# Gate sums taken from the value products: w_gate applied to v, head by head, in place of the transposed output rows

## What is computed

```python
    scores = scale * np.matmul(q, k.transpose(0, 1, 3, 2))      # B=2, H=8, S=768, D=64
    keep = is_sink | in_window                                   # 4 sinks, window of 128
    a = np.exp(scores - max) ;  a = a / (sum + 1e-09)
    return np.matmul(a, v).astype(np.float32)
...
    x = attn_out.transpose(0, 2, 1, 3).reshape(B * S, H * D)     # 1536 x 512
    logits = x @ w_gate                                          # w_gate: 512 x 8
    # greedy assignment by logits, cap = N // E, then relu(x @ w1[e]) @ w2[e] by expert
    # at last ((y @ w_a) * (y @ w_b)) @ w_out
```

## Time and profile before

| | us |
|---|---|
| median of 3 runs | 622.15 (621.51 to 623.23) |
| the profiled execution | 621.72 |
| its span in the trace | 620.0 |
| PE busy | 581.6 |
| DVE busy | 416.3 |
| POOL busy | 337.3 |
| ACT busy | 316.3 |

### The profile page before, as it was taken

One profiled execution on the slowest core, in us unless ns is written; L12 is line 12 of the kernel. 1 busy time (PEld: TensorE's weight loads), 2 busy tenths in 40 slices (PEclk: granted clock), 3 DMA queues, 4 the chain that ended last, 5 costly groups with the idle time before them and its releaser, 6 DMA issues.

```text
span 620.0 us, 11120 instructions
## 1 busy us (share of the span) xinstructions
PE 581.6 (94%) x3816; PEld 526.1 (85%) x3818; DVE 416.3 (67%) x1079; ACT 316.3 (51%) x767; POOL 337.3 (54%) x408
## 2 busy tenths in 40 slices
PE   8999999994359999999999999999999999999996
PEld 4888778863239999999999999999999999999984
DVE  3889669847845776767985566847746646656663
ACT  4798569742304776667775444534534424424410
POOL 7211101100012502268886999997997898687623
PEclk9999999996559999999999999999999999999999
DMA  9995050505022865667663222312222323210102
GB/s 188 267 221 122 19 178 27 162 27 162 1 53 69 282 213 202 208 222 247 214 214 101 78 78 69 102 45 93 69 68 69 121 87 99 68 49 22 34 1 102
DMA packets 87650, 72.12 MB, mean 116 GB/s; under 512 B 39976, under 2 KB 74792, under 8 KB 87592
## 3 DMA queue, kind: packets, MB, share of 16 engines
q1 hardware_dynamic: 83888, 64.64, 35.1%
q0 software_dynamic: 1920, 6.29, 3.0%
q10 hardware_dynamic: 1784, 0.44, 0.4%
HBM read 65.08 MB, written 6.29 MB: 115 GB/s over the span
## 4 chain that ended last, share of the span: by engine, by line
PE 82%; DVE 10%; POOL 3%; ACT 2%; issue 2%; DVEq 0%; ACTq 0%
PE psum L1885 12%; PE psum L1964 9%; PE psum L1967 9%; PE psum L1966 9%; PE psum L1886 6%; PE psum L1879 5%; PE psum L1880 5%; PE psum L1687 5%; PE psum L1878 5%; PE psum L1649 4%; PE psum L1670 3%; PE psum L1626 2%; DVE above L1339 2%; PE psum L1621 1%; DVE w_lo L1102 1%
## 5 line engine op out<-in xcount | busy, mean ns | idle before, releaser
L780 POOL TENSOR_TENSOR w_lo<-w_raw,w_hi 128x512 fp32r<-128x512 f32 x96 | 109.6, 1176 | 24.1 <-ACT w_hi L995 24.1
L1885 PE MATMUL psum<-h_hl,w_hi 128*128 128x384 f32 x256 | 75.5, 363 | 1.0 <-POOL w_lo L703 0.5
L1885 PE MATMUL psum<-x_hl,w_hi 128*128 128x384 f32 x256 | 74.0, 361 | 0.3 <-DVE x_hl L1474 0.3
L1966 PE MATMUL psum<-x_hl,w_hi 128*128 128x384 f32 x216 | 72.2, 334 | 0.0
L863 ACT ACTIVATE w_hi<-w_raw 128x1024 fp32r<-128x1024 f32 (+1 forms) x72 | 69.1, 960 | 0.0
L1102 DVE TENSOR_TENSOR w_lo<-w_raw,w_hi 128x1024 fp32r<-128x1024 f32 x44 | 65.1, 1479 | 0.0
L1886 PE MATMUL psum<-x_hl,w_lo 128*128 128x192 f32 x256 | 64.2, 251 | 0.0
L1602 DVE TENSOR_TENSOR o_acc<-psum,o_acc 128x512 f32<-128x512 f32 x60 | 41.2, 690 | 34.2 <-PE psum L1880 34.0
L1886 PE MATMUL psum<-h_hl,w_lo 128*128 128x192 f32 x256 | 64.2, 251 | 0.0
L688 POOL CAST p_sink<-p_sb 128x16 fp32r<-128x16 f32 x40 | 8.1, 203 | 98.8 <-ACT p_sb L884 78.3
L1964 PE MATMUL psum<-x_hl,w_hi 128*128 128x384 f32 x168 | 56.3, 335 | 0.4 <-POOL w_lo L780 0.4
(11 more groups left out here) (237 smaller groups left out, 1528.1 us busy)
## 6 DMA issues: line engine op xcount, KB each, us to landing
w_raw<-in_moe_w_dram SPq DMA_DIRECT2D x32, 1024.0 KB, 5.5
w_raw<-in_moe_w_a_dram SPq DMA_DIRECT2D x12, 512.0 KB, 3.6
w_raw<-in_moe_w_b_dram SPq DMA_DIRECT2D x12, 512.0 KB, 3.5
w_raw<-in_moe_w_out_dram SPq DMA_DIRECT2D x12, 512.0 KB
k_raw<-in_k_dram SPq DMA_DIRECT2D x16, 192.0 KB, 4.4
v_sb<-in_v_dram SPq DMA_DIRECT2D x16, 192.0 KB, 3.7
xs_scratch<-x_rows SPq DMA_DIRECT2D x8, 384.0 KB, 3.4
q_raw<-in_q_dram SPq DMA_DIRECT2D x14, 192.0 KB, 4.4
```

Of the source, the lines that this page charges most:

```text
L780: return nc.gpsimd.tensor_tensor(out_t, t, hi_t.bitcast(f32), ALU.subtract)
L1885: nc.tensor.matmul(bk[:, 0:2 * CAP], lhs_hi, rhs_both, start=first, stop=False)
L1966: nc.tensor.matmul(o, w_h, t_lo[:, t, :], start=False, stop=False, skip_group_check=True)
```

## The change

A head's output row is a weighted sum of rows of v. So its part of the logits is the same weighted sum of v times that head's 64 rows of w_gate. For each group, w_gate's part is applied to v before the values are used: v's six blocks are transposed (three and three, new side kind `v`), ACT copies them to vT, seven products with wg (`gates`) give eight columns for each head and block (and for the sink rows), and DVE copies those next to v, in front of the first head and behind the second (v_sb is now 144 wide for a pair and not 128). The value product of a head then has 72 columns, the sink product 144, and x_rows keeps 8 gate sums beside each head's 64 outputs. `sum_logits` adds the 8 heads' sums with one reduction for each batch (batch 1 in two pieces). The row transposes, the gate and logits jobs, LAST_GATE and the products behind the last step go. The sink values are rounded group by group after their gate columns are there. Group 0's v is transposed and multiplied at the start, in the places of three and of six fillers. The product that sums absum moves from behind the last step into step 44.

```diff
-                jobs += [(t + 4, 0, "rows", g, 0)]
                 if g + 1 < PAIRS:
-                    jobs += [(t + 7, 0, "rows", g, 1)]
-                    if g % NPAIR == NPAIR - 1:
-                        jobs += [(t + 5, 1, "gate", g, 0), (t + 6, 1, "logits", g, 0),
-                                 (t + 8, 1, "gate", g, 1), (t + 9, 1, "logits", g, 1)]
-            last = PAIRS - 1
-            return sorted(jobs + [(STEPS_A, 0, "rows", last, 1), (STEPS_A, 1, "rows", last, 2)])
+                    jobs += [(t + 3, 1, "v", g + 1, 0), (t + 4, 0, "v", g + 1, 1), (t + 4, 1, "gates", g + 1, 0)]
+            return sorted(jobs)
...
-        SINKS_AT = {1: (1, 2, 3), 2: (4, 5, 6, 7)}
+        SINKS_AT = {NBLK * g + NBLK - 1: g + 1 for g in range(PAIRS - 1)}
...
+            def keep_sinks(g):
+
+                b, pr = divmod(g, NPAIR)
+                if g == 0:
+                    pool.wait_ge(sink_in, 16 * 6)
+                    pool.wait_ge(first_gates_kept, 1)
+                else:
+                    pool.wait_ge(side_done, side_number("gates", g, 0) + 1)
+                nc.gpsimd.tensor_copy(v_sink[:, b, pr, :], sink_raw[:, b, pr, :]).then_inc(sink_rounded, 1)
...
+            def keep_vT(bk, half):
+
+                if half == 0:
+                    for h in range(2):
+                        rows = slice(h * D, (h + 1) * D)
+                        nc.scalar.activation(sinkT[rows, :].rearrange("p (z n) -> p z n", n=2 * NSINK)[:, 0::4, NSINK * h:NSINK * (h + 1)],
+                                             bk[rows, 0:NSINK].unsqueeze(1).to_broadcast([D, 3, NSINK]), ACT.Copy)
+                return nc.scalar.activation(vT[:, half * HS:(half + 1) * HS], bk[:, 0:HS], ACT.Copy)
...
+            for half in range(2):
+                act.wait_ge(first_v, half + 1)
+                keep_vT(bank[2 + half], half).then_inc(first_vT, 1)
             exps(0)
...
+            def keep_gates(bk, g):
+
+                for z, kept in enumerate(value_gates(g % NPAIR)):
+                    nc.vector.tensor_copy(kept, bk[:, 0:NBLK * 2 * E].rearrange("p (i n) -> p i n", n=2 * E)[:, :, z * E:(z + 1) * E])
+                for z, kept in enumerate(sink_gates(g)):
+                    at = NBLK * 2 * E + z * E
+                    op = nc.vector.tensor_copy(kept, bk[0:SINK_ROWS, at:at + E])
+                return op
+
+            def sum_logits(first, last):
+
+                dve.wait_ge(x_kept, (NPAIR - 1 + last // NBLK * NPAIR) * NBLK + last % NBLK + 1)
+                heads = x_rows[:, first:last + 1, :, :].rearrange("p c r (u e) -> p c e r u", e=E)[:, :, :, :, 0::PW // E - 1]
+                return nc.vector.tensor_reduce(out=L[:, first:last + 1, :], in_=heads, axis=AX.XY, op=ALU.add)
...
+                if t == STEPS_A - 1:
+                    sum_logits(NBLK, NCH - 2).then_inc(logits_kept, 1)
+            sum_logits(NCH - 1, NCH - 1).then_inc(logits_kept, 1)
...
-                                                v_sb[:, pr, i - 1 + blk, h, :], start=(h == 0 and blk == t0),
+                        hw = slice(h * PW // 2, (h + 1) * PW // 2)
+                        last = nc.tensor.matmul(o[:, hw], pT[:, t % 2, blk, h, :],
+                                                v_sb[:, pr, i - 1 + blk, hw], start=(h == 0 and blk == t0),
...
+            def turn_v(bk, pr, half):
+
+                for jj in range(3):
+                    op = nc.tensor.transpose(bk[:, jj * P:(jj + 1) * P], v_sb[:, pr, 3 * half + jj, E:PW - E], ident[:])
+                return op
+
+            def gates(bk, pr):
+
+                for i in range(NBLK):
+                    nc.tensor.matmul(bk[:, i * 2 * E:(i + 1) * 2 * E], vT[:, i * P:(i + 1) * P], wg[:, pr, :],
+                                     start=(i == 0), stop=True, skip_group_check=True)
+                return nc.tensor.matmul(bk[0:SINK_ROWS, NBLK * 2 * E:(NBLK + 1) * 2 * E], sinkT[:], wg[:, pr, :],
+                                        start=False, stop=True, skip_group_check=True)
...
-            spinning(3, bank[0])
+            pe.wait_ge(v_in[0], 32)
+            for half in range(2):
+                turn_v(bank[2 + half], 0, half).then_inc(first_v, 1)
             scores(0)
+            pe.wait_ge(first_vT, 2)
             scores(1)
...
-            spinning(6, bank[6])
+            pe.wait_ge(wg_in, 32)
+            gates(bank[6], 0).then_inc(first_gates, 1)
...
-            pe.wait_ge(sums_kept, 1)
-            for i in range(3):
-                nc.tensor.matmul(bank[2][:, 2 * E * i:2 * E * (i + 1)], LT2[:, i * P:(i + 1) * P],
-                                 ident[0:2 * E, 0:2 * E], start=(i == 0), stop=False, skip_group_check=True)
+                if t == STEPS_A - 4:
+                    pe.wait_ge(abs_ready, 1)
+                    pe.wait_ge(side_done, SIDES)
+                    nc.tensor.matmul(bank[7][:, 0:1], ones[:], absum[:], start=True, stop=True).then_inc(abs_summed, 1)
```

More of the change, by code:

```diff
@@ L544, in _ @@
                     sp.wait_ge(consts, 2)
[L545 removed]
+                    for hh in range(2):
+                        sp.dma_start(wg[hh * D:(hh + 1) * D, :, hh * E:(hh + 1) * E], wg_v[hh]).then_inc(wg_in, 16)
             for u in range(2):
@@ L696, in _ @@
                     pool.wait_ge(sink_split, no + 1)
-                    for g in SINKS_AT[t]:
-                        lower_sinks(g)
+                    keep_sinks(SINKS_AT[t])
             def split_lo(n, u):
@@ L723, in _ @@
                 nc.gpsimd.indirect_dma_start(
-                    out=x_rows[:, place(st), :], out_offset=None, in_=xs_dram[:, :],
+                    out=x_got[:, place(st), :], out_offset=None, in_=xs_dram[:, :],
                     in_offset=bass.IndirectOffsetOnAxis(ap=ids[:, st:st + 1], axis=0)).then_inc(xg_in[st], 16)
@@ L914, in side_jobs @@
                     else:
[L915 to L920 removed]
+                        keep_vT(bank[7], half).then_inc(side_done, 1)
             def round_ahead(t):
@@ L1200, in _ @@
             invert_den(1)
+            dve.wait_ge(sink_in, 16 * 6)
+            dve.wait_ge(first_gates, 1)
+            keep_gates(bank[6], 0).then_inc(first_gates_kept, 1)
             for t in range(1, STEPS_A + 1):
@@ L1696, in values @@
                 last.then_inc(o_ready, 1)
-            def last_gate(half, blk):
-                both = wg[:, blk, 1 - half:3 - half, :].rearrange("p z e -> p (z e)")
-                return nc.tensor.matmul(bank[7][0:2 * E, 0:HS], both, xT[:, blk, half * HS:(half + 1) * HS],
-                                        start=(half == 0 and blk == 0), stop=(blk == KD - 1))
+            def turn_v(bk, pr, half):
[8 more added lines that the diff above has]
+                                        start=False, stop=True, skip_group_check=True)
             def side_jobs(t, late):
@@ L1710, in side_jobs @@
                         pe.wait_ge(first_lo, 4)
[L1711 removed]
+                    pe.wait_ge(side_done, job)
                     b, pr = divmod(g, NPAIR)
                     hs = slice(half * HS, (half + 1) * HS)
[L1714 to L1730 removed]
+                    if kind == "v":
+                        if half == 0:
+                            pe.wait_ge(v_in[pr], 32 * (b + 1))
+                        op = turn_v(bank[7], pr, half)
+                    elif kind == "gates":
+                        op = gates(bank[7], pr)
                     else:
@@ L1866, in turn_x @@
                 for t in range(KD):
-                    last = nc.tensor.transpose(bank[bk][:, t * P:(t + 1) * P], x_rows[:, place(s), t * P:(t + 1) * P],
+                    last = nc.tensor.transpose(bank[bk][:, t * P:(t + 1) * P], x_got[:, place(s), t * P:(t + 1) * P],
                                                ident[:])
```

151 lines of the change are left out of this document (51 added, 100 removed).

## The result

The changed kernel takes **659.0 us** (median of 4 runs, 650.3 to 671.5), the kernel before it 622.0 (4 runs, 621.5 to 623.2). The ratio is 1.049 (95% interval 1.042 to 1.055), from the two runs of the changed kernel with the highest granted clock; the other two are longer still. So the sign of the prediction was right and its size was not: 626.0 us was forecast, with a range that ended at 629.5. The profiled execution took 654.78 us.

A forecast was written before the change was run, and what follows sets the result against it. The prediction took TensorE's instruction list to bound the attention stage. It summed 22.0 us coming and 17.7 us going to +4.3 us, on 621.72 us of profiled execution: 626.0 us, range 621.3 to 629.5.

The forecast's parts named there:

- The step that failed: Attention stage: a group takes 14.37 us with TensorE busy throughout at clock 1.00, so TensorE's instruction list sets the pace.
- The gate products: TensorE, seven groups: seven f32 matmuls make 14 passes bound by weight loads, 0.112 us each, 1.57 us a row.
- v's first half waits for q_lo: Step 6g+3: v's transposes wait until q_hi and q_lo have read bank 7; TensorE idle 0.45 us a group.
- The second wait: Step 6g+4: gate products wait for ACT's second vT half; with 0.05 us for pTs, TensorE idle 0.35 us a group.
- the term for weights rounded ahead: ACT's weight rounding falls between vT's halves in three groups (steps 9, 15, 33): 0.45 us each, 1.3 us in all.
- 72 columns cost nothing: Value products: 72 columns in place of 64 add 0 us, since weight loads set the pace; upper bound 4.9 us.
- The tail: From the last x_rows tile to m: 2.56 us becomes 0.83 us, so 1.7 us go.
- The start: Six v transposes wait for v before the first scores, which start at 9.5 us: 1.1 us added (0.5 to 1.8).
- a block that moves as a whole: Router and experts behind the attention stage start when the logits are there and move together, with no change priced.
- The rivals: No difference, 622.3 us (0.19); faster, 618.7 (0.10); much slower, 630.2, and 72 columns paid in full, 630.9 (together 0.12).
- much slower: Attention loop: ACT, held for v, delays exponentials; 0.6 us more a group, 630.2 us; chance 0.12 shared with the columns rival.
- The rival on columns: Value products: 72 columns instead of 64 paid in full, +4.9 us, 630.9 us; chance 0.12 shared with much slower.

The follow-up runs named there:

- the kernel with wide passes: The changed kernel with each gate product streaming all four pairs' 64 gate columns, not 16; also called the wide form; 630.5 us median, 1.0135 times the kernel before.
- the kernel with rows of 28: The kernel before plus two times seven idle f32 products of 16 columns (28 passes) in step 6g+4 of seven groups; 674.3 us, 1.0854.
- the first case: Changed kernel with 64-column gate products and v sets away from q, then v's first transposes moved behind scores(1); 625.3 us, against 625.7 without that move.
- the second: Changed kernel with 32-column gate products spread over three steps, six side sets in six steps, start transposes moved; 621.4 us against 622.1 for the kernel before.

## Why the prediction was wrong

**The step that failed stands in its first part**: a group takes 14.37 us "at a granted clock of 1.00". It was true of the kernel before. Every term of the sum then took it over as a constant, with no rival in which the clock falls, though the change took wide work out (30 passes of 384 columns) and put 98 passes of 16 in (and 14 more at the start). The gate products were priced at 1.57 us a row and cost 1.49; what they did to the clock cost 24 us in the profiled run, over five times the whole sum of +4.3. What the runs show in place of the constant is a stage at a mean clock of 0.82 (16.53 to 174.07), with 58.0 us at half clock, 0.41 us lost for each. The sentence "not the columns but the loads set the pace" was right, and it should have raised the question what an array does that mostly loads.

**The steps at full clock held.** They are to be read in the kernel with wide passes, and in the changed kernel's stretches at 1.00:
- 14 gate passes: 64.01 to 65.50, 1.49 us; 1.57 forecast.
- v's first half waits for q_lo. The prediction took the wait from start to start: 1.79 us from q to the next user of the bank where it would be 1.34, so 0.45. In the six groups with wide passes it is 1.79 to 2.06 us, a wait of 0.45 to 0.72. (The idle times in brackets, 0.28 to 0.55, count from the modelled end of the matmul before.)
- The second wait (0.35 forecast) is there in ordinary groups, in two parts that the list of waits is too coarse to name. With wide passes, the sink product starts 0.95 us behind the value products (0.81 without a wait), and the gate products 0.38 behind it (0.15 for what follows elsewhere): 0.37 us. The second part is the one for ACT's vT, as the weight loads of the changed kernel name it:

```profile
27.32 1.41 PEld L1732 LDWEIGHTS psum<-wg,vT 128*128 128x128 f32 x12 [0.19 <-ACT vT L913]
```

- The three waits of 0.47 us for pTs are the term for weights rounded ahead: they stand in the groups of steps 9, 15 and 33, the three that the prediction named. There the two parts come to 0.90 us (1.48 and 0.38 from start to start); 0.35 + 0.45 were forecast.
- 72 columns cost nothing. From 19.11 to 19.92, 0.81 us for a set of eight passes:

```profile
19.11 1.01 PE L1712 MATMUL psum<-v_sb,pT 128*128 128x72 f32 x8
19.92 0.32 PE L1719 MATMUL psum<-v_sink,pTs 72*128 72x144 f32 x1
```

- The tail: the last x_rows tile to m in 0.91 us; 0.83 forecast, 2.56 before:

```profile
173.16 0.31 DVE L1175 TENSOR_TENSOR x_rows<-psum,rden 128x144 f32<-128x144 f32 x1 [0.69 <-PE psum L1719]
173.50 0.27 DVE L1192 TENSOR_REDUCE L<-x_rows 128x8 f32<-128x64 f32 x1
...
174.07 0.20 DVE L1284 TENSOR_REDUCE m<-L 128x12 f32<-128x96 f32 x1
```

- The start: v lands later than assumed, and scores(0) start at 10.02, not 9.5; 8.70 before:

```profile
9.21 0.88 PE L1726 MATMUL psum<-ident,v_sb 128*128 128x128 f32 x6 [1.03 <-DMA v_sb<-in_v_dram]
10.02 0.33 PE L1671 MATMUL psum<-k_hi,q_hi 64*128 64x128 f32 x2
```

**Terms that were too small.** The kernel with wide passes took 631.1 us where 626.0 were forecast for that clock. Of the 5.1 us, 2.0 lie in the six groups shown above (104.2 us against 6 x 16.75 + 1.7): an ordinary one takes 16.8 to 17.05, and one with weights rounded ahead 17.6 to 17.9, where I had added 0.6 and it is 0.9. 1.1 are the start: the first k set comes 1.8 us later than before, and the sinks' transpose behind it, which waits 0.5 us for POOL, 2.2 later, where 1.1 was forecast for all. 1.7 are the way from m to the end (479.1 against 477.5 us), which I had called a block that moves as a whole. The last 0.3 was not traced. So even with the clock held the change costs 9.4 us in the profiled run where 4.3 were forecast, and the median of 630.5 lies beyond the range: the forecast was low before the clock came into it. (The range's lower end is 626.0 - 4.9 = 621.1 by its own terms, not 621.3.)

**The rivals.** None of them came. The one called "much slower" had the right sign and a mechanism (ACT's exponentials late) that no row shows. Chance for slower was 0.71. With the clock held, slower is what these terms give; that the measured kernel took 37 us more by the medians, and not 4.3, is for the larger part the clock's. The rival on columns stood at 630.9, close to the 630.5 of the kernel with wide passes, by chance: 72 columns cost nothing, as the rows above show.

The Trainium skill, "TensorE: Matmul & The Clock Gate", section "What's actually happening", says that the throttled state is the default and that activity releases it. The kernel before agrees behind its attention stage: with PE busy for 5.25 us from 155.00 to 170.50 it is granted 0.50, and with 15.18 us from 186.00 to 201.50 it is granted 1.00. Its start does not show a throttled default: the first 2 us stand at 1.00 with PE busy for 0.46. And a stage in which PE is busy for 98% of the time, with rows of thin passes in it (173.82 of 176.51 us), was granted 0.84. The Trainium skill's section "HAM oscillation — how this bites in real kernels" puts the falls down to idle gaps between bursts of matmuls. Here the measurement decides: the longest idle time of PE in the changed kernel's stage is 0.55 us, the waits stayed when the passes were widened and the falls went, and a fall came behind 13.66 us without any wait.

## What to carry to other kernels

Price a change to TensorE's list twice, once by the time of its passes and once by what they do to the clock: a granted clock of 1.00 in the profile of before is a result of that kernel's mix of passes, not a property of the stage. Where f32 passes are bound by their weight loads, columns are nearly free up to 128 (0.111 to 0.116 us a pass at 128, 0.111 at 16), so a thin product can stream idle columns at almost no cost; and thin products that must stay thin are better placed one or two at a time between wide ones than in one row. When a kernel's times scatter by some per cent, compare the mean clock of each run first.

## What had not been expected of the hardware

- TensorE's granted clock halved while PE was busy all the time: behind 14 passes of 16 columns (four rows of eight, with one or two idle times of 0.28 to 0.55 us ahead of them; a fifth row with idle times of 0.28 and 0.47 us had none), and inside or right behind each of seven rows of 28 such passes in a kernel without added waits. With 64 columns it never did in the profiled run, with the same waits, and the mean clock of all 4 runs is that of the kernel before.
- A us at half clock cost 0.41 us in this stage, not 0.5 (some 0.45 in the kernel with rows of 28: 176.51 - 127.76 - 196 x 0.116 = 26.0 us for 58.0), and over the four runs of the changed kernel the time follows the clock: against the wide form (631.1 us, 0.964), the run at 0.894 has 97 us more at half clock (2 x 0.106 x 669.8 - 2 x 0.036 x 629.4) and takes 40.5 us longer, 0.42 for each.
- A stage that is done 0.8 us earlier, or 2.1, handed on only 0.1 and 1.0 of it. The clock of the routing went from 0.59 to 0.56 in the first case and stayed at 0.59 in the second, where the cause is open.
